# Experts worked in units of 256 rows, with the first weight matrix as the stationary operand

## The reference

```python
for b in range(B):
    prev_e = -1
    for s in range(S):
        fresh_e = int(np.argmax(logits[b, s]))
        if s == 0 or local_gate[b, s] < 0.5:
            e = fresh_e
        else:
            e = prev_e if prev_e >= 0 else fresh_e
        prev_e = e
        ...
        h = np.maximum(x[b, s] @ w1[e], 0.0)
        out[b, s] = p[e] * (h @ w2[e])
```

## Time and profile before

| | |
|---|---|
| runs before | 830.54 us median of 3 (829.87 to 830.96) |
| profiled execution | span 834.7 us; no own time is given beside it |
| PE busy over the span | 712.2 us, 85% |
| stage of the experts | from about 376 to 602 us of the span |
| chunks in it | 16, two for each expert |
| period of one expert | 26.80 us |

### The profile page before, as it was taken

How to read it: one execution, slowest core, us unless ns; L and a number is a source line. 1 busy time by engine, 2 the same in 40 slices (tenths; PEclk the granted TensorE clock), 3 DMA queues, 4 the chain that set the end, 5 groups by cost and what they waited for, 6 DMA issues and landing times. The chain is left out here.

```text
span 834.7 us, 11494 instructions
## 1 busy us (share of the span) xinstructions
PE 712.2 (85%) x3946; PEld 618.6 (74%) x3947; DVE 391.7 (47%) x573; ACT 296.8 (36%) x420; POOL 285.9 (34%) x212
## 2 busy tenths in 40 slices
PE   2899999999999989407999999999564679999997
PEld 1799999999999979405777777777453457888885
DVE  7666566665666401512343443433268996111111
ACT  2334443344433413203445354543235754111100
POOL 2123232232322215353354544533175755111100
PEclk9999999999999965557999999999877899999998
DMA  5034533354333107333655556441161001111000
GB/s 133 1 98 149 142 99 97 97 153 139 97 97 97 61 23 281 101 151 97 232 178 200 187 189 215 164 151 39 51 196 69 0 1 36 65 64 64 25 25 25
DMA packets 50075, 89.52 MB, mean 107 GB/s; under 512 B 17280, under 2 KB 17280, under 8 KB 50048
## 3 DMA queue, kind: packets, MB, share of 16 engines
q1 hardware_dynamic: 48128, 82.87, 31.2%
q0 software_dynamic: 1920, 6.29, 2.3%
HBM read 63.98 MB, written 25.17 MB: 107 GB/s over the span
## 5 line engine op out<-in xcount | busy, mean ns | idle before, releaser
L361 PEld LDWEIGHTS pv<-v_ones,probs 128*128 128x128 f32 x1152 | 146.7, 198 | 1.2 <-ACT probs L232 1.2
L361 PE MATMUL pv<-v_ones,probs 128*128 128x65 f32 x1152 | 144.0, 277 | 0.9 <-ACT probs L232 0.9
L839 POOL TENSOR_TENSOR w_lo<-stage,w_hi 128x1024 fp32r<-128x1024 f32 x28 | 90.0, 3217 | 107.3 <-ACT w_hi L834 107.1
L321 DVE TENSOR_REDUCE row_max<-ring 128x1 f32<-128x768 f32 x96 | 86.5, 951 | 9.7 <-PE ring L391 8.7
L232 ACT ACTIVATE probs<-ring 128x768 f32<-128x768 f32 x96 | 71.2, 812 | 23.3 <-PE ring L424 22.0
L879 DVE TENSOR_TENSOR ht_lo<-ht_ps,ht_hi 128x512 fp32r<-128x512 f32 x32 | 22.1, 691 | 106.2 <-ACT ht_hi L868 106.2
L157 POOL TENSOR_TENSOR k_lh<-k_raw,k_aug 64x768 fp32r<-64x768 f32 x16 | 32.8, 2052 | 105.2 <-DVE k_aug L272 105.2
L391 PE MATMUL ring<-k_aug,q_aug 96*128 96x384 f32 x192 | 57.6, 386 | 8.0 <-DVE row_max L321 6.8
L934 PE MATMUL down<-w_hi,ht_hi 128*128 128x512 f32 x128 | 52.9, 413 | 9.0 <-DVE ht_lo L879 9.0
L834 ACT CAST w_hi<-stage 128x1024 fp32r<-128x1024 f32 x56 | 58.7, 1048 | 0.0
L1144 ACT CAST m_xt_hi<-m_tp 128x512 fp32r<-128x512 f32 x24 | 13.9, 579 | 123.7 <-PE m_tp L1306 123.7
(11 more groups left out here) (190 smaller groups left out, 1381.2 us busy)
## 6 DMA issues: line engine op xcount, KB each, us to landing
stage<-in_w SPq DMA_DIRECT2D x64, 512.0 KB, 6.4
x_slots<-zeros SPq DMA_DIRECT2D x7, 1024.0 KB, 5.4
y_slots<-zeros SPq DMA_DIRECT2D x7, 1024.0 KB, 5.2
q_raw<-in_qT SPq DMA_DIRECT2D x32, 192.0 KB, 5.3
k_raw<-in_kT SPq DMA_DIRECT2D x32, 192.0 KB, 4.6
x_all<-x_slots SPq DMA_DIRECT2D x18, 256.0 KB, 2.7
wt_raw<-in_w_tok SPq DMA_DIRECT2D x6, 768.0 KB, 4.3
y_slots<-x_all SPq DMA_DIRECT2D x16, 256.0 KB, 6.8
```

What stands on the lines that cost most here:

```text
L321: nc.vector.tensor_reduce(row_max[:, j:j + 1], ring[j % 3][:, :, 0:HALF], AX.XY, ALU.max).then_inc(s_max, 1)
L361: last = nc.tensor.matmul(pv[:, t * (D + 1):(t + 1) * (D + 1)], probs[:, k, t * P:(t + 1) * P], v_ones[p][:, k, :], start=k == 0, stop=k = ...
L839: name.tensor_tensor(w_lo[w][:, r, :], stage[:, r, :], w_hi[w][:, r, :].bitcast(F32), ALU.subtract).then_inc(done, 1)
```

## The change

Rows are handled in units of 256 (`UNIT`), at least one for each expert. In the first layer the roles of the operands are exchanged: a 128x128 block of `w1` is stationary and the transposed rows move, 256 columns at a time. The inner activations come out transposed, so the transposes of them, `hid` and `ht_ps` are gone: ACT's relu writes `ht_hi` directly, and DVE makes `ht_lo` from the same PSUM tile by one instruction (maximum with zero, less the high part). The second layer keeps its form and is run for each half of the unit (`down[0]`, `down[1]`). Between the two halves stand the eight transposes of the next unit's rows. `x_in`, `y_out` are buffers of their own; `x_all` is freed before the experts, and lies at the other end of SBUF. Each load and store has 512 KB. The slots in DRAM grow from 3584 to 4480 rows, so the 14 clearing DMAs have 1.25 MB each, and were of 1 MB.

The core of the diff:

```diff
-MIN_CHUNKS = 2
-MAX_CHUNKS = NC + E * MIN_CHUNKS - MIN_CHUNKS
+UNIT = 2 * P
+MIN_UNITS = 1
+MAX_UNITS = NC // 2 + E * MIN_UNITS - MIN_UNITS
...
-    up = [ps(f"up{n}", [P, 512]) for n in range(2)]
-    ht_ps = [ps(f"ht_ps{n}", [P, 512]) for n in range(2)]
-    xt_ps = ps("xt_ps", [P, 512])
-    down = ps("down", [P, 512])
+    up = [ps(f"up{n}", [P, 2, UNIT]) for n in range(4)]
+    xt_ps = [ps(f"xt_ps{n}", [P, 2, UNIT]) for n in range(2)]
+    down = [ps(f"down{n}", [P, 512]) for n in range(2)]
...
+        def unit(g, e, w, first, more):
+            if first and more and not (isinstance(e, int) and e + 2 >= E):
+                for r in range(NP):
+                    free_piece(e + 1, r)
+                    load_piece(sp, w1, w2, stage, s_st, e + 2, r)
             sp.wait_ge(s_xt, g + 2)
             load_x(g + 2)
-            sp.wait_ge(s_y, g + 1)
+            sp.wait_ge(s_y, 2 * g + 2)
...
+        def unit(g, e, w, first, more):
+            for n in range(4):
+                act.wait_ge(s_up, 4 * g + n + 1)
+                nc.scalar.activation(ht_hi[:, 2 * n:2 * n + 2, :], up[n][:], ACT.Relu).then_inc(s_hh, 1)
+                if first and more:
+                    piece_high(act, e + 1, 1 - w, 2 * n)
+                    piece_high(act, e + 1, 1 - w, 2 * n + 1)
+            x_high(g + 1)
...
+        def unit(g, e, w, first, more):
+            for n in range(4):
+                dve.wait_ge(s_hh, 4 * g + n + 1)
+                at = slice(2 * n, 2 * n + 2)
+                nc.vector.scalar_tensor_tensor(ht_lo[:, at, :], up[n][:], 0.0, ht_hi[:, at, :].bitcast(F32), ALU.max,
+                                               ALU.subtract).then_inc(s_hl, 1)
+                if first and more:
+                    piece_low(dve, nc.vector, s_wlv, e + 1, 1 - w, 2 * n)
+            x_low(g + 1)
...
-            run(first).then_inc(s_up, 1)
-            run(second[:8])
-            transpose_h(g, 0)
-            run(second[8:]).then_inc(s_up, 1)
-            pe.wait_ge(s_hh, 2 * g + 1)
-            pe.wait_ge(s_hl, 2 * g + 1)
-
-            out = down_products(w)
-            run(out[:4])
-            transpose_h(g, 1)
-            run(out[4:12])
-            transpose_x(g + 1)
...
+            pe.wait_ge(s_xl, 2 * g + 2)
+            for f in range(KF):
+                for k in range(KD):
+                    for n, (a, b) in enumerate(PARTS):
+                        last = nc.tensor.matmul(up[f // 2][:, f % 2, :], (w_hi, w_lo)[b][w][:, k, f * P:(f + 1) * P],
+                                                (xt_hi, xt_lo)[a][:, k, :], start=k == 0 and n == 0,
+                                                stop=k == KD - 1 and n == 2)
+                if f % 2 == 1:
+                    last.then_inc(s_up, 1)
+            for j in range(2):
+                if j == 1:
+                    transpose_x(g + 1)
+                for f in range(KF):
+                    if j == 0 and f % 2 == 0:
+
+                        pe.wait_ge(s_hl, 4 * g + f // 2 + 1)
+                    for n, (a, b) in enumerate(PARTS):
+                        last = nc.tensor.matmul(down[j][:], (ht_hi, ht_lo)[a][:, f, j * P:(j + 1) * P],
+                                                (w_hi, w_lo)[b][w][:, NP // 2 + f // 2, (f % 2) * DM:(f % 2 + 1) * DM],
+                                                start=f == 0 and n == 0, stop=f == KF - 1 and n == 2)
+                last.then_inc(s_down, 1)
```

More of the change, by code:

```diff
@@ L661, in _ @@
                                           ALU.mult, ALU.add))
[L662 removed]
+        link(nc.vector.tensor_scalar(count[:], upto[:, :, NC - 1], float(UNIT - 1), None, ALU.add))
         link(nc.vector.tensor_copy(count_i[:], count[:]))
[L664 to L665 removed]
+        link(nc.vector.tensor_scalar(count_i[:], count_i[:], 8, None, ALU.logical_shift_right))
+        link(nc.vector.tensor_scalar(chunks[:], count_i[:], float(MIN_UNITS), None, ALU.max))
         link(nc.vector.tensor_tensor_scan(chunk_end[:], ones_e[:], chunks[:], 0.0, ALU.mult, ALU.add))
@@ L731, with experts @@
 KF = F // P
-BATCHED = 4
-def experts(nc, ctx, w1, w2, x_slots, y_slots, ident, chunk_tab, weights, x_all, load_theta):
+def experts(nc, ctx, w1, w2, x_slots, y_slots, ident, chunk_tab, weights, load_theta):
     def sb(name, shape, dt=F32):
@@ L745, in experts @@
     stage, w_hi, w_lo, s_st, s_wh, s_wlv, s_wlp = weights
[L747 to L753, removed]
-    up = [ps(f"up{n}", [P, 512]) for n in range(2)]
-    ht_ps = [ps(f"ht_ps{n}", [P, 512]) for n in range(2)]
-    xt_ps = ps("xt_ps", [P, 512])
-    down = ps("down", [P, 512])
+    x_in = sb("x_in", [P, 2, DM])
+    y_out = sb("y_out", [P, 2, DM])
+    xt_hi = sb("xt_hi", [P, KD, UNIT], F32R)
+    xt_lo = sb("xt_lo", [P, KD, UNIT], F32R)
+    ht_hi = sb("ht_hi", [P, KF, UNIT], F32R)
+    ht_lo = sb("ht_lo", [P, KF, UNIT], F32R)
+    up = [ps(f"up{n}", [P, 2, UNIT]) for n in range(4)]
+    xt_ps = [ps(f"xt_ps{n}", [P, 2, UNIT]) for n in range(2)]
+    down = [ps(f"down{n}", [P, 512]) for n in range(2)]
     s_xin = sem("e_xin")
@@ L774, in table, with over_experts @@
     def table(engine, e):
-        n = engine.value_load(chunk_tab[0:1, 0, bass.ds(e, 1)], min_val=MIN_CHUNKS, max_val=MAX_CHUNKS)
-        base = engine.value_load(chunk_tab[0:1, 1, bass.ds(e, 1)], min_val=0, max_val=MAX_CHUNKS - MIN_CHUNKS)
+        n = engine.value_load(chunk_tab[0:1, 0, bass.ds(e, 1)], min_val=MIN_UNITS, max_val=MAX_UNITS)
+        base = engine.value_load(chunk_tab[0:1, 1, bass.ds(e, 1)], min_val=0, max_val=MAX_UNITS - MIN_UNITS)
         return n, base
-    def over_experts(engine, prologue, chunk):
+    def over_experts(engine, prologue, unit):
         prologue()
@@ L786, in one @@
             n, base = table(engine, e)
[L787 to L791, removed]
+            unit(base, e, w, True, more)
+            with engine.If(n > MIN_UNITS):
+                with engine.Fori(MIN_UNITS, n) as c:
+                    unit((base + c).with_bounds(min_val=MIN_UNITS, max_val=MAX_UNITS - 1), e, w, False, False)
         with engine.Fori(0, E // 2 - 1) as i:
@@ L817, in prologue @@
             load_theta(sp)
-        def chunk(g, e, w, part):
+        def unit(g, e, w, first, more):
[3 more added lines that the diff above has]
+                    load_piece(sp, w1, w2, stage, s_st, e + 2, r)
             sp.wait_ge(s_xt, g + 2)
             load_x(g + 2)
[L823 to L826, removed]
-            sp.wait_ge(s_y, g + 1)
-            sp.dma_start(y_rows[bass.ds(g, 1), :, :].rearrange("a p d -> (a p) d"), y_out).then_inc(s_out, 16)
-        over_experts(sp, prologue, chunk)
+            sp.wait_ge(s_y, 2 * g + 2)
+            sp.dma_start(y_rows[bass.ds(g, 1), :, :, :].rearrange("a p j d -> (a p) j d"), y_out[:]).then_inc(s_out, 16)
+        over_experts(sp, prologue, unit)
     def piece_high(act, e, w, r):
@@ L855, in _, with x_high @@
     def _(act):
+        def x_high(g):
+            act.wait_ge(s_xt, g + 1)
+            for n in range(2):
+                nc.scalar.copy(xt_hi[:, 2 * n:2 * n + 2, :], xt_ps[n][:]).then_inc(s_xh, 1)
         def prologue():
[L857 to L872, removed]
@@ L874, in _ @@
-        over_experts(act, prologue, chunk)
+            x_high(0)
+        def unit(g, e, w, first, more):
[6 more added lines that the diff above has]
+            x_high(g + 1)
+        over_experts(act, prologue, unit)
@@ L876, in _, with x_low @@
     @block.vector
     def _(dve):
-        def low(dst, src_ps, hi, done):
-            nc.vector.tensor_tensor(dst, src_ps, hi.bitcast(F32), ALU.subtract).then_inc(done, 1)
-        def prologue():
[L882 to L895, removed]
+        def x_low(g):
+            for n in range(2):
+                dve.wait_ge(s_xh, 2 * g + n + 1)
+                at = slice(2 * n, 2 * n + 2)
+                nc.vector.tensor_tensor(xt_lo[:, at, :], xt_ps[n][:], xt_hi[:, at, :].bitcast(F32),
+                                        ALU.subtract).then_inc(s_xl, 1)
@@ L897, in chunk @@
             dve.wait_ge(s_out, 16 * g + 16)
-            nc.vector.tensor_copy(y_out, down[:]).then_inc(s_y, 1)
-        over_experts(dve, prologue, chunk)
+            for j in range(2):
+                dve.wait_ge(s_down, 2 * g + j + 1)
+                nc.vector.tensor_copy(y_out[:, j, :], down[j][:]).then_inc(s_y, 1)
+        over_experts(dve, prologue, unit)
     @block.tensor
     def _(pe):
+        PARTS = ((0, 0), (0, 1), (1, 0))
         def transpose_x(g):
@@ L906, in transpose_x @@
             for k in range(KD):
-                last = nc.tensor.transpose(xt_ps[:, k * P:(k + 1) * P], x_in[:, k * P:(k + 1) * P], ident[:])
+                for j in range(2):
+                    last = nc.tensor.transpose(xt_ps[k // 2][:, k % 2, j * P:(j + 1) * P],
+                                               x_in[:, j, k * P:(k + 1) * P], ident[:])
             last.then_inc(s_xt, 1)
@@ L911, in prologue, with unit @@
             transpose_x(0)
```

(29 more changed lines are left out.)

29 lines of the change are left out of this document (15 added, 14 removed).

## The result

| | median | runs |
|---|---|---|
| before | 830.57 us | 829.05 to 835.59, 20 runs |
| changed | 836.27 us | 829.10 to 841.12, 20 runs |

The ratio of changed to before is 1.0053 (95% interval 1.0033 to 1.0074). Run ten times more later, beside another set of runs of before, the changed kernel had 832.3 us and a ratio of 0.9994 (0.9968 to 1.0021). So it is half a per cent slower or the same, and not 15 us faster.

A forecast was written before the change was run, and what follows sets the result against it. PE was taken to bound the experts' stage, by its work and not its clock. The terms -14.4 - 11.9 + 7.6 + 3.1 = -15.6 us took the median from 830.5 to 815 us, range 803 to 822.

The forecast's parts named there:

- Two of the 1.25 MB clearings ride behind the loads of each pair of heads, where the DMA share is 0.36: Attention's DMA queue: the larger clearings were listed as moved or added at nearly nothing.
- The first layer's products: Experts: 384 products of 512 columns become 768 of 256 at 0.123 us each, a loss of 7.6 us.
- both rivals on it: First layer: load not covered by its product, 866 us, 4 in 100; load and product alternate, 892 us, 2 in 100.
- The transposes: Experts: 48 groups of four go, eight groups of eight stay at 0.89 us each; a gain of 14.4 us.
- The wait between the layers: Experts: PE's 16 waits of 0.744 us for `ht_lo` go, a gain of 11.9 us.
- The hand-over: PE's passage to the next expert: 0.70 us, 0.47 over the pace; no gain from it in the sum.
- My third rival: Experts: next weights come late from POOL, PE waits 2 us in each of seven units; 829 us, 4 in 100.
- The last 0.4 us of an expert: Second layer: a pace slightly over 0.2263 us, which the change leaves.
- The period: Time of one expert on PE: to fall from 26.8 to 24.3 us.
- The ends: Before the first and after the last expert: larger load and store, more transposes, one more copy; a loss of 3.1 us.

The follow-up runs named there:

- the run with 1 MB: Changed kernel with the attention's clearing DMAs back at 1 MB each, the rest cleared once after the last loads: 809.5 us, ratio 0.975.
- The run with the pieces in the first chunk: Kernel before, with all eight pieces of the next expert's weights split in the first chunk of an expert: 885.5 us, ratio 1.063.
- the run with the new places alone: Kernel before, with only `zeros`, `x_all` and `w_route` moved to the other end of SBUF: 830.8 us, ratio 0.9986.
- the kernel before with the early place: Kernel before, its 1 MB clearings issued ahead of SP's wait for the products with v: 822.9 us, ratio 0.988.
- the run of both remedies: Changed kernel with clearings of 1 MB, issued ahead of SP's wait for the products with v: 803.6 us, ratio 0.964.

## Why the prediction was wrong

The step that failed is the sentence "Two of the 1.25 MB clearings ride behind the loads of each pair of heads, where the DMA share is 0.36". I priced it at nothing. They ride ahead of the next head's q and k, since SP stands still between, until the products with v are done. And the share of busy DMA engines was the wrong thing to ask: it is 0.4 in a stretch in which DVE waits for a load in nearly every head, and PE for DVE. The list of waits of 0 to 325 us shows both, first before and then in the changed kernel:

```profile
DVE k_aug L272 <- DMA k_raw<-in_kT: 74.7, 13, 6.1
PE ring L391 <- DVE row_max L321: 6.8, 14, 1.4
...
DVE k_aug L272 <- DMA k_raw<-in_kT: 79.0, 13, 6.9
PE ring L391 <- DVE row_max L321: 10.5, 19, 1.4
```

The row of PE was there to be read before the change: a later load had no slack. The cost was 12.0 us of wait and 12.4 of clock. Without it, by the run with 1 MB, the kernel has 809.5 us: inside the range, 5 us under the 815 forecast. The 5 us are the experts': their terms gave 18.7 us (14.4 + 11.9 - 7.6), and in that run they took 191.2 us, 24 less than before.

The other steps, term by term, in the changed kernel's rows:

- **The first layer's products.** From 437.66 to 440.18 are 21 products, 0.120 us each, where I had taken 0.123. 768 x 0.120 = 92.2 us, a loss of 5.3 and not 7.6. The load stays hidden under 256 columns, and both rivals on it fall. The rule on loads of the Trainium skill ("TensorE: Matmul & The Clock Gate", "Part 3: Packing small matmuls — row/col tiling") would have given 0.22, by the prediction's estimate; the trace does not agree.
- **The transposes.** From 445.54 to 446.88 lie eight transposes and two products, 1.34 us; less two paces, 0.89. As predicted.
- **The wait between the layers.** 440.18 to 440.30, 0.12 us, is the pace. The 11.9 us are gone as predicted.
- **The hand-over.** I left 0.47 us in each expert. It is gone in six of seven: 451.87 to the next first product at 452.10. The first, 427.69 to 428.69, takes 1.00 us. The run with the pieces in the first chunk showed that the 0.47 was the wait for POOL. In a unit POOL's last piece is done at 446.94, 5 us ahead of the expert's end, where before it was done at 436.46, 0.3 us ahead of the next product. 7 x 0.47 - 0.77 = 2.5 us more gain. My third rival feared that these weights come late; it had the sign wrong.
- **The last 0.4 us of an expert.** I took them for a slow pace in the second layer, "which the change leaves". Most of them went too: before, the second product behind each wait starts 0.31 us after the first and not 0.23 (443.51 and 443.82, behind a wait for `ht_lo`), and with the 23 waits some 2 us are gone.
- **The period** is 23.3 us (24.3 predicted), and the experts' gain 26.3 us, before the ends.
- **The ends.** Transposes to first product 3.97 us, where it was 2.61: 1.4, as predicted (1.5). From the attention's last mark to these transposes 87.3 us, where the run with the new places alone has 86.5: 0.8, which is what the larger first load was priced at. From the last product to the mixing's first transpose 10.07 us and before 9.39: 0.7 (0.8 predicted). Together 2.9 (3.1 predicted). The other 2.8 us behind the experts are no constant price of the change: what lies behind the experts takes 236.8 to 241.2 us in seven profiles of kernels with the new experts, and 237.8 to 238.1 in four with the old.

With equal attention the change is worth 19.3 us, some 4 less than these rows add up to (26.3 - 2.9 = 23.4). Most of that lies in the experts: 215.8 us in the kernel before with the early place, 192.8 in the run of both remedies, a gain of 22.9. Of the seven hand-overs of the latter two take 1.86 and 2.64 us, in both together 4.0 over the pace, and nothing in the profile releases them. The six other profiles of the changed experts have none, one or two such hand-overs, 0.5 to 1.8 us over the pace. One in the run with 1 MB, on PE:

```profile
544.04 0.39 PE L938 MATMUL down<-w_hi,ht_lo 128*128 128x512 f32 x1
546.10 0.38 PE L925 MATMUL up<-xt_hi,w_hi 128*128 128x256 f32 x1 [1.67 <-issue]
```

All of them are the first hand-over or, as here, the last: the first lies in the first turn of the loop over experts, the last behind the loop, and the ones between are at the pace. What PE waits for there stays open: that its code arrives late would fit, but no run here tests it.

## What to carry to other kernels

A change in one stage may have its price in another: list every transfer whose size moves with a constant, look up what stands behind it on its queue, and ask whether that is waited for now. The DMA share of 0.36 said nothing of that here; the row of the wait did. Work that nobody waits for in time, like clearing, belongs behind the loads that are waited for: this alone took 10 us off the kernel before (ratio 0.988), and together with the change 28 us (ratio 0.963).

A stationary operand exchanged for a moving one can take out transposes and the wait for them. Here the price was 5.3 us of longer products, against 14.4 us of transposes and 11.9 of waits, and the loads stayed hidden: the closest start 0.11 us apart, and the products 0.12.

## What the hardware showed that I had not expected

- The granted clock of PE fell to 0.50, the lower level of 1.2 GHz, inside a stretch in which no wait of PE was longer than 0.80 us. It stayed at 1.00 once products that nobody reads stood in these waits, and the whole was 14 us faster (832.3 to 818.0 on one chip).
- DVE's subtraction of 128 x 1024 took 1.35 us in the mean before, and 3.0 in the run in which DVE and POOL both split their four pieces without a pause.
- A wait can cost twice through the clock: 256 KB more in one kind of transfer cost 8.6 us, with the clock at 1.00, and the next 256 KB 24.4, of which 12.4 are the fall of the clock.
